# Loads, a list and a wait around the experts' program of a three-stage kernel on one Trainium2 core

## The reference, cut to what matters

```python
def _attn_ref(r, k, v, w, u):            # 4 x 8 x 768 x 48
    for t in range(S):
        kt, vt, rt = (k[:, :, t], v[:, :, t], r[:, :, t])
        cur = np.einsum('bhd,bhe->bhde', u[None] * kt, vt)
        y[:, :, t] = np.einsum('bhd,bhde->bhe', rt, state + cur)
        state = w[None, :, :, None] * state + np.einsum('bhd,bhe->bhde', kt, vt)

def _moe_ref(x, w_skip, w_gate, w1, w2): # x 3072 x 384, 8 experts, 1024 wide
    xc = x[x @ w_skip > 0]
    logits = xc @ w_gate
    e_idx = np.argmax(logits, axis=1)    # gate_w: softmax of the logits at e_idx
    for e in range(E):
        mask = e_idx == e
        y[mask] = gate_w[mask, None] * (np.maximum(xc[mask] @ w1[e], 0.0) @ w2[e])
    out[x @ w_skip > 0] = xc + y

def _moe2_ref(x, w1, w2, w3, w_out):
    return (((x @ w1) * (x @ w2)) @ w3) @ w_out
```

## Time and profile before

| what | us |
|---|---|
| median of three executions | 644.26 (644.2 to 646.89) |
| the profiled execution | 643.48 |
| its span, first to last instruction | 641.7 |
| TensorE busy | 606.6 |
| VectorE, ScalarE, GpSimd busy | 297.0, 215.5, 148.3 |

### The profile page before, as it was taken

One profiled execution on the slowest core, in us unless ns is written; L12 is line 12 of the kernel. 1 busy time (PEld: TensorE's weight loads), 2 busy tenths in 40 slices (PEclk: granted clock), 3 DMA queues, 4 the chain that ended last, 5 costly groups with the idle time before them and its releaser, 6 DMA issues. The chain is left out here.

```text
span 641.7 us, 17460 instructions
## 1 busy us (share of the span) xinstructions
PE 606.6 (95%) x7377; PEld 536.9 (84%) x7377; DVE 297.0 (46%) x456; ACT 215.5 (34%) x383; POOL 148.3 (23%) x183
## 2 busy tenths in 40 slices
PE   7799988798899999999979999999999999999997
PEld 6698888655699999999858898898888888888886
DVE  5578877268178776778212232132223223223222
ACT  2244444324256655455142232122113113123112
POOL 7477776225004444431122000000000000000000
PEclk9799999799999999999999999999999999999999
DMA  7589889464165667773040002002002001001001
GB/s 145 111 173 189 184 184 241 126 241 149 42 238 206 225 240 260 265 264 119 21 148 1 1 28 72 0 1 99 1 1 99 0 1 50 1 1 49 1 0 50
DMA packets 103801, 67.77 MB, mean 106 GB/s; under 512 B 79252, under 2 KB 97816, under 8 KB 103760
## 3 DMA queue, kind: packets, MB, share of 16 engines
q1 hardware_dynamic: 75824, 57.88, 29.8%
q10 hardware_dynamic: 26144, 4.74, 3.9%
q0 software_dynamic: 1792, 4.58, 1.9%
HBM read 55.92 MB, written 12.19 MB: 106 GB/s over the span
## 5 line engine op out<-in xcount | busy, mean ns | idle before, releaser
L1508 DVE TENSOR_TENSOR gl_g_sb<-gl_a_sb,gl_pab 128x512 f32<-128x512 f32 x48 | 33.0, 687 | 186.3 <-ACT gl_a_sb L1485 186.3
L1428 PE MATMUL gl_pab<-gl_xT_hi,wm_lo 128*128 128x512 f32 x288 | 112.9, 392 | 0.0
L1428 PE MATMUL gl_pab<-gl_xT_lo,wm_hi 128*128 128x512 f32 x288 | 112.8, 392 | 0.0
L1428 PE MATMUL gl_pab<-gl_xT_hi,wm_hi 128*128 128x512 f32 x288 | 112.2, 389 | 0.0
L1485 ACT ACTIVATE gl_a_sb<-gl_pab 128x512 f32<-128x512 f32 x48 | 28.7, 597 | 184.0 <-PE gl_pab L1428 184.0
L1428 PEld LDWEIGHTS gl_pab<-gl_xT_hi,wm_lo 128*128 128x128 f32 x288 | 54.0, 188 | 11.4
L1428 PEld LDWEIGHTS gl_pab<-gl_xT_hi,wm_hi 128*128 128x128 f32 x288 | 54.1, 188 | 10.6 <-DVE gl_xT_lo L1515 0.3
L1428 PEld LDWEIGHTS gl_pab<-gl_xT_lo,wm_hi 128*128 128x128 f32 x288 | 54.0, 188 | 10.5
L1286 DVE TENSOR_TENSOR ew_w_lo<-ew_w_in,ew_w_hi 128x768 fp32r<-128x768 f32 x32 | 46.6, 1457 | 17.8 <-ACT ew_w_hi L1248 17.0
L1189 PE MATMUL ex_ph<-ex_xT_hi,ew_w_hi 128*128 128x224 f32 x192 | 52.9, 275 | 0.0
L1189 PE MATMUL ex_ph<-ex_xT_hi,ew_w_lo 128*128 128x224 f32 x192 | 52.7, 274 | 0.0
(11 more groups left out here) (203 smaller groups left out, 1217.2 us busy)
## 6 DMA issues: line engine op xcount, KB each, us to landing
ew_w_in<-in_moe_w SPq DMA_DIRECT2D x16, 1536.0 KB, 7.9
w_in<-in_moe_w SPq DMA_DIRECT2D x14, 512.0 KB, 7.2
k_in<-in_k SPq DMA_DIRECT2D x48, 96.0 KB
v_in<-in_v ACTq DMA_DIRECT2D x48, 96.0 KB, 3.4
r_in<-in_r SPq DMA_DIRECT2D x48, 96.0 KB
xbuf<-x_nat SPq DMA_DIRECT2D x24, 192.0 KB
gl_x_in<-xbuf SPq DMA_DIRECT2D x12, 384.0 KB, 4.2
out<-gl_o_sb SPq DMA_DIRECT2D x12, 384.0 KB, 2.4
```

The lines of the kernel that those rows point to most:

```text
L1428: m = pe.matmul(p_ab[f % 2][w][:, :], a[:, w * KD + k, cols], b[t.slot][:, k, :], start=(k == 0 and n == 0), stop=(k == KD - 1 and n == 2))
L1508: dve.tensor_tensor(g_sb[f % 2][:, :], a_sb[f % 2][:, :], p_ab[f % 2][1][:, :], ALU.mult).then_inc(s_g, 1)
```

## The change

Three things are changed, and one follows from them.

- In `Fold.product` the wait for `s_Wout` goes from i to i - 1: product i no longer waits until product i - 1 was taken, but until product i - 2 was, the last one in its bank.
- In the routing block TensorE's second list of slots, with its two waits, moves from behind product 3 to behind turn 6.
- The loads of the gated stage's first two x tiles (four transfers of 384 KB) move from the gated block to the end of SP's list in the experts' block. There SP waits for the last split of w1, for a new semaphore `s_over` that GpSimd increments behind its overflow loop, and for all scatters. The wait for the scatters in the gated block goes.
- The x tiles of the gated stage now lie in the buffer `w1_in`, of the same size, which is allocated outside the experts' scope; the gated stage's own x tiles go.

```diff
@@ class Fold, product @@
         if 0 in quarters:
             wait(pe, self.s_Tout, 2 * i + 2)
-            wait(pe, self.s_Wout, i)
+            wait(pe, self.s_Wout, i - 1)
@@ routing, TensorE @@
                 fold.turn(pe, 4, p_T[0])
                 fold.product(pe, 3, p_W[1])
+                fold.turn(pe, 5, p_T[1])
+                fold.product(pe, 4, p_W[0])
+                fold.turn(pe, 6, p_T[0])
                 pe.wait_ge(s_table, 1)
                 pe.wait_ge(s_gval, 3)
                 for t in range(NT):
                     m = pe.matmul(p_list[:, 2 * NSL:5 * NSL], oh_lo[:, t, :], vals[:, t, 2:5, :].rearrange("p v s -> p (v s)"),
                                   start=(t == 0), stop=(t == NT - 1))
                 m.then_inc(s_list, 1)
-                fold.turn(pe, 5, p_T[1])
-                fold.product(pe, 4, p_W[0])
-                fold.turn(pe, 6, p_T[0])
                 fold.turn(pe, 7, p_T[1])
                 fold.product(pe, 5, p_W[1], (0, 1))
@@ new @@
+class GatedInputs:
+    def __init__(self, sem, w1_in, TOK, DM):
+        self.TOK = TOK
+        self.x_in = [w1_in[:, :, :].rearrange("p k f -> p (k f)")[:, i * TOK // P * DM:(i + 1) * TOK // P * DM].rearrange("p (i d) -> p i d", d=DM)
+                     for i in range(2)]
+        self.s_x = [[sem(f"x{i}{h}") for h in range(2)] for i in range(2)]
+
+    def load(self, sp, xbuf, slot, n):
+        TOK = self.TOK
+        for h in range(2):
+            sp.dma_start(self.x_in[slot][:, 2 * h:2 * h + 2, :],
+                         xbuf[bass.ds(n * TOK + h * TOK // 2, TOK // 2), :].rearrange("(i p) d -> p i d", p=P)).then_inc(self.s_x[slot][h], 16)
@@ experts, SP @@
                 overflow(sp, body, n)
+                sp.wait_ge(s_w1lo, E * NG)
+                sp.wait_ge(s_over, 1)
+                for s in s_out:
+                    sp.wait_ge(s, 32 * env["n_scattered"])
+                for i in range(2):
+                    env["gated_x"].load(sp, xbuf, i, i)
@@ experts, GpSimd @@
                 overflow(pool, body, n)
+                pool.sem_inc(s_over, 1)
@@ gated layers, SP @@
                 def load(t):
+                    if isinstance(t.c, int) and t.num() < 2:
+                        return
                     wait(sp, s_T, t.num(2, -2))
-                    for h in range(2):
-                        sp.dma_start(x_in[t.slot][:, 2 * h:2 * h + 2, :],
-                                     xbuf[bass.ds(t.num(TOK, h * TOK // 2), TOK // 2), :].rearrange("(i p) d -> p i d", p=P)).then_inc(s_x[t.slot][h], 16)
+                    gx.load(sp, xbuf, t.slot, t.num())
-                for s in env["s_scattered"]:
-                    sp.wait_ge(s, 32 * env["n_scattered"])
@@ program @@
         attention(nc, env, r, k, v, w, u, xbuf)
+        w1_in = sb("w1_in", [P, KD, FM])
+        env["gated_x"] = GatedInputs(scope(c, "gl_")[1], w1_in, 4 * P, DM)
         with ExitStack() as ce:
-            env["experts"] = ExpertInputs(*scope(ce, "ew_"), moe_w1, moe_w2)
+            env["experts"] = ExpertInputs(*scope(ce, "ew_"), moe_w1, moe_w2, w1_in)
```

More of the change, by code:

```diff
@@ L952, in rows, with __init__ @@
         return min(P, self.ROOM - i * P)
-    def __init__(self, sb, sem, w1, w2):
+    def __init__(self, sb, sem, w1, w2, w1_in):
         E, DM, FM = w1.shape
@@ L957, in __init__ @@
         self.w1, self.w2, self.NG = w1, w2, KF // 2
-        self.w1_in, self.w2_in = sb("w1_in", [P, KD, FM]), sb("w2_in", [P, KF, DM])
+        self.w1_in, self.w2_in = w1_in, sb("w2_in", [P, KF, DM])
         self.w1_hi, self.w1_lo = sb("w1_hi", [P, KD, FM], F32R), sb("w1_lo", [P, KD, FM], F32R)
@@ L1045, in experts @@
         s_H, s_hhi, s_hlo = sem("H"), sem("hhi"), sem("hlo")
-        s_Y, s_new = sem("Y"), sem("new")
+        s_Y, s_new, s_over = sem("Y"), sem("new"), sem("over")
         s_wmin, s_wmhi, s_wmlo = [sem(f"wmin{i}") for i in range(2)], sem("wmhi"), env["s_wmlo"]
@@ L1343, in gated_layers @@
         p_o += [env["p_pair"][:, i, :] for i in range(2)]
-        x_in = [sb(f"x_in{i}", [P, NI, DM]) for i in range(2)]
         xT_hi = [sb(f"xT_hi{i}", [P, KD, TOK], F32R) for i in range(2)]
@@ L1351, in gated_layers @@
         o_sb = [sb(f"o_sb{i}", [P, NI, DM]) for i in range(2)]
-        s_x = [[sem(f"x{i}{h}") for h in range(2)] for i in range(2)]
+        gx = env["gated_x"]
+        x_in, s_x = gx.x_in, gx.s_x
         s_T, s_xhi, s_xlo = sem("T"), sem("xhi"), sem("xlo")
```

## The result

The changed kernel takes **634.58 us** (median of four executions, 631.32 to 636.58); the kernel before took 644.46 beside it. The ratio is 0.985 [0.981, 0.9891].

The account below looks back on a forecast made before the run. TensorE, busy for 95% of the span, bounds the kernel, so only its holes can be won. 0.8 + 3.0 + 0.8 + 2.5 = 7.1 us takes the median of 644.26 to 637.2 us, range 636.0 to 640.4.

Parts of the forecast that it names:

- Part 1, the bank: Products wait for the bank two back: product 2 and the last product each start 0.8 us earlier.
- the far ends: Upper, start-to-start values of the terms: 0.92, 3.07, 0.84 and 2.55 us, 7.4 us together.
- Part 2, the list: Routing: the second list goes behind the turn of chunk 6, so turn 5 starts earlier, worth 3.0 us.
- The cover behind turn 6: Routing: the list's 1.26 us fit into the wait before turn 7, with 0.17 us left over.
- (d): Something unseen fixes the first expert's start, so routing's 3.8 us are lost: 641.0 us; chance 0.05.
- Part 3, the loads: Hand-over to the gated stage: first x rows loaded inside the experts' program, transposes earlier, worth 2.5 us.
- Rival (a): Barrier opens only after SP's four loads land, losing 1.4 to 3.3 us: 638.6 to 640.5 us; chance 0.10.
- (c): Barrier waits for loads after slow scatters and TensorE's clock falls: 646.8 us, slower than before; chance 0.02.
- The sum: Routing and hand-over gains added, 0.8 + 3.0 + 0.8 + 2.5 = 7.1 us.
- the base and the edge of the range: Kernel before taken as 644.26 us; low end 636.0, the sum's far end less what runs differ by.
- The rule on the clock: Idle gaps halve TensorE's clock: held true at 117 us, not at 325 us; the sum stays unchanged.

Follow-up runs that it names:

- e7: Second list of slots moved ahead of turn 6 instead of behind it, against the changed kernel; 635.08 us, ratio 0.9893 to the kernel before.
- e8: SP waits for its four x loads to land before going to the barrier, against the changed kernel; 640.94 us, ratio 0.9979 to the kernel before.
- e2: The kernel before, executed again without any edit; 642.78 us, ratio 0.9986.
- e3: The kernel before with only the x tiles placed in w1_in and the new semaphores, loads still in the gated block; 643.96 us, ratio 0.9993.
- e9: 40 unread transposes put into attention's TensorE hole, against the changed kernel; 635.63 us, ratio 0.9894 to the kernel before.

## Why the prediction was right, and where it was wrong

**Part 1, the bank: right, the far ends.** Product 2 won 0.92 us and the last product 0.84, where I took 0.8 each. A hole is worth its start-to-start length, since the matmul that follows really starts that much earlier; the idle row is short by the modelled tail. I knew this, worked "from start to start", and then took values between it and the idle rows.

**Part 2, the list: right.** 3.08 against 3.0. The cover behind turn 6 holds with the 0.17 us foreseen (turns 6 and 7 are 2.31 us apart in both kernels), and e7 shows what stands there without it. The first expert's start followed in full (routing is 4.06 us shorter), so (d) is out.

**Part 3, the loads: right.** 2.55 against 2.5. The issues begin 2.6 us behind the scatter's start (2.5 foreseen), and no first transpose waits. Rival (a) is out by 317.98 against 319.7; e8 shows that a held barrier would have cost both parts of the price in (c): waiting, and 2.8 us of clock where 3.3 were foreseen (117.7 to 124.5 us, which it read as 6.7, is 6.8).

**The sum: mis-sized by 0.4 us**, 7.5 against 7.1, which is the sum of the values chosen below the far ends. The far ends give 7.4, and only these are start to start.

**The step of the prediction that failed is the base and the edge of the range**: "The median of the runs shown is 0.78 above it, 644.26", and a low end of 636.0 as "the far end of the sum, less what runs differ by". Three executions were taken for the kernel's level, and 0.9 us for what an execution may differ (636.9 to 636.0). Larger samples put the kernel before at 643.62 (29 executions), 642.71 (25) and 643.18 (15), 0.6 to 1.6 us lower, with single executions 8 to 10 us apart (the longest of the first and of the second left out). A stretch that the change doesn't touch, attention, runs from 128.22 to 135.54 us in the twelve traces. No term of the sum stood for it, though the trace of before had 17 us at 1.2 GHz in attention (25 to 33, 117 to 125 and 127 to 132 us), of which the prediction read the second. Take 79 executions of the kernel before (these three samples and e2, without the same two) and set the span against the time lost to the clock, (1 - mean granted clock) x span: a fitted line gives a span of 636.1 + 0.64 x lost, and this takes the standard deviation from 2.1 to 1.4 us. For the 16 executions of the changed kernel it is 626.2 + 0.86 x lost. At the same 7.5 us lost they are 8.2 us apart, against 7.5 by the touched stretches. The 0.7 us between are two standard errors of the fit, so whether the change gives more than these stretches show stays open.

From 643.2, the mean of those three medians, the far ends (7.4, or the 7.5 measured) would have given 635.8 or 635.7, with some 1.4 us to either side as the standard error of a median of four executions (1.25 x 2.2 / 2, for a deviation of 2.2 us). 634.58, 635.35 and 634.74 lie inside that. Of the 2.6 us between 637.2 and 634.58, 0.4 are thus the sum and 1.1 the base; the last 1.1 are no more than what four executions leave open.

**The rule on the clock.** The Trainium skill (TensorE: Matmul & The Clock Gate, Why this matters for your kernels) says that idle gaps between bursts halve the clock; I held that it didn't bear on 325 us, where the granted clock was 1.00. e3's 0.50 there, behind nearly the same holes, goes the page's way, though its row speaks of longer gaps than these, and the kernel before's 1.00 doesn't. So moving the loads may also take away a fall that some executions have: of the five traces with the loads in the old place one shows it, of the six with the loads moved and the barrier not held none. How many executions have it no run here shows.

## What to carry to other kernels

Price a hole from start to start, and use that value; the idle row is a lower bound only. Before the range is drawn, ask which stretches outside the change vary, and by how much: the granted clock of several executions, or one more trace of the kernel before, would have shown 4.5 us in attention (133.57 and 129.03). A transfer may be left in flight across a block's barrier as long as no engine's own list waits for it, and work that needs no new input fits well behind an operation whose successor must wait for a copy.

## What the hardware showed that was not expected

- TensorE was through the barrier at a block's end at 317.98 us with at least one load in flight until 319.7; a wait of SP's own for the same loads held it for 4.48 us (e8).
- The same hole of 2.7 to 2.8 us on TensorE was followed by 6.8 us at 1.2 GHz in one execution (2.81) and by none in another (2.74, e2).
- The clock fell at the hand-over in e3 and not in the kernel before, with nearly the same holes (1.66 and 0.27 us against 1.62 and 0.51).
- For the second to the seventh expert one VectorE split of w2 takes 2.23 to 3.85 us instead of 0.96 (changed kernel and e9), the one that runs beside GpSimd's split of 2.4 us.
